# Turning a tile's hidden values in the middle of the results of the tile in front

## What is computed

```python
def _moe2_ref(x, expert_emb, tau, w1, w2):
    xn = x / (np.linalg.norm(x, axis=-1, keepdims=True) + 1e-06)
    en = expert_emb / (np.linalg.norm(expert_emb, axis=-1, keepdims=True) + 1e-06)
    logits = xn @ en.T / tau
    expert_idx = np.argmax(logits, axis=1)
    ...
    for e in range(E):
        mask = expert_idx == e
        h = np.maximum(x[mask] @ w1[e], 0.0)
        out[mask] = gate_w[mask, None] * (h @ w2[e])
```

## Time and profile before

| | us |
|---|---|
| median of 3 runs (lowest, highest) | 835.03 (833.4, 835.28) |
| the profiled execution | 834.27 |
| its span, first to last instruction | 832.3 |
| mean granted TensorE clock | 0.999 |
| TensorE busy (matmuls) | 814.6 (98%) |
| VectorE busy | 564.4 (68%) |
| ScalarE busy | 438.8 (53%) |
| GpSimd busy | 203.3 (24%) |

### The profile page before, as it was taken

One profiled execution on the slowest core, in us unless ns is written; L12 is line 12 of the kernel. 1 busy time (PEld: TensorE's weight loads), 2 busy tenths in 40 slices (PEclk: granted clock), 3 DMA queues, 4 the chain that ended last, 5 costly groups with the idle time before them and its releaser, 6 DMA issues.

```text
span 832.3 us, 18049 instructions
## 1 busy us (share of the span) xinstructions
PE 814.6 (98%) x5633; PEld 763.7 (92%) x5633; DVE 564.4 (68%) x1315; ACT 438.8 (53%) x924; POOL 203.3 (24%) x286
## 2 busy tenths in 40 slices
PE   6999999999999999999999999999999999999997
PEld 6899999999999999999999999999889998898896
DVE  6879788879889878879888855635452512545463
ACT  6675564464464465465456435553552533565563
POOL 5611111122103013103113001303343323334433
PEclk9999999999999999999999999999999999999999
DMA  9975432155242141232210001414531513376392
GB/s 215 206 150 130 77 68 39 34 92 69 51 73 34 31 84 33 39 83 38 39 34 30 1 16 30 171 47 128 168 124 40 185 47 100 134 259 201 92 315 66
DMA packets 165307, 78.56 MB, mean 94 GB/s; under 512 B 135486, under 2 KB 153253, under 8 KB 165090
## 3 DMA queue, kind: packets, MB, share of 16 engines
q1 hardware_dynamic: 156402, 64.81, 32.3%
q0 software_dynamic: 4544, 10.85, 4.0%
q10 hardware_dynamic: 4272, 1.82, 0.9%
HBM read 112.90 MB, written 11.63 MB: 150 GB/s over the span
## 4 chain that ended last, share of the span: by engine, by line
PE 85%; SPq 7%; DVE 3%; issue 2%; ACT 1%; DMA 1%; POOL 0%; DVEq 0%; ACTq 0%; POOLq 0%
PE bank L1065 22%; PE bank L1044 21%; PE bank L1117 13%; PE bank L1153 13%; SPq L458 3%; PE bank L1134 3%; PE bank L970 2%; PE bank L937 2%; PE bank L998 2%; PE bank L993 2%; SPq L483 1%; PE bank L1099 1%; PE bank L978 1%; SPq L471 1%; SPq L490 1%
## 5 line engine op out<-in xcount | busy, mean ns | idle before, releaser
L1044 PE MATMUL bank<-xhl,WRh 128*128 128x384 f32 x768 | 219.0, 339 | 0.7 <-DVE WRl L1715 0.5
L1044 PEld LDWEIGHTS bank<-xhl,WRh 128*128 128x128 f32 x768 | 141.3, 188 | 1.2 <-issue 1.2
L1411 ACT COPY gw<-bank 128x384 f32<-128x384 f32 x128 | 61.6, 481 | 152.3 <-PE bank L1044 150.9
L1065 PE MATMUL bank<-WRh,gh 128*128 128x384 f32 x384 | 135.8, 354 | 0.0
L1044 PE MATMUL bank<-xhl,WRl 128*128 128x384 f32 x384 | 130.0, 339 | 0.0
L1065 PE MATMUL bank<-WRh,gl 128*128 128x384 f32 x384 | 129.8, 338 | 0.0
L1065 PE MATMUL bank<-WRl,gh 128*128 128x384 f32 x384 | 129.7, 338 | 0.0
L1734 DVE TENSOR_TENSOR gl<-gw,gh 128x384 fp32r<-128x384 f32 x128 | 72.2, 564 | 56.6 <-ACT gh L1417 52.7
L1417 ACT CAST gh<-gw 128x384 fp32r<-128x384 f32 x128 | 65.2, 510 | 76.7 <-DVE gw L1727 64.4
L1727 DVE SCALAR_TENSOR_TENSOR gw<-gw 128x384 f32<-128x384 f32 x128 | 75.7, 592 | 31.3 <-ACT gw L1411 30.9
L1902 DVE TENSOR_TENSOR hl<-bank,hh 128x512 fp32r<-128x512 f32 x56 | 36.1, 686 | 84.0 <-ACT hh L1452 83.7
(11 more groups left out here) (199 smaller groups left out, 1639.7 us busy)
## 6 DMA issues: line engine op xcount, KB each, us to landing
stage<-in_moe_w_dram SPq DMA_DIRECT2D x96, 768.0 KB
Kn<-in_k_dram SPq DMA_DIRECT2D x24, 192.0 KB, 3.4
Vn<-in_v_dram SPq DMA_DIRECT2D x24, 192.0 KB, 3.2
x_moe<-x2s SPq DMA_DIRECT2D x24, 192.0 KB, 2.0
Rn<-in_r_dram SPq DMA_DIRECT2D x21, 192.0 KB, 2.8
wraw<-in_moe_w_out_dram SPq DMA_DIRECT2D x4, 768.0 KB, 7.4
eraw<-in_moe_w_dram SPq DMA_DIRECT2D x4, 768.0 KB, 8.9
Wn<-in_w_dram SPq DMA_DIRECT2D x152, 16.0 KB, 1.8
```

The lines of the kernel that those rows point to most:

```text
L1044: mm = pe.matmul(bank[F_BANK[n % 2]][:, 0:GN], win(t_)[:, f // 4, k_, cols], xhl[G % 2][:, a, k_, :], start=(k_ == 0 and n_ == 0), stop=(k ...
L1065: mm = pe.matmul(bank[O_BANK[i]][:, 0:DM], a[:, z, cols], wout(t_)[:, f, :], start=(f == 0 and n_ == 0), stop=(f == FT - 1 and n_ == 2))
L1411: act.copy(gw[:, n % 2, :], bank[F_BANK[n % 2]][:, 0:GN]).then_inc(s_g0, 1)
```

## The change

On TensorE the results of the tile in front are cut in two halves and the turns of tile j are put between them. The results of tile 0 (`start_moe`) and of the last tile keep their place. Which tile writes `s_o2`, and when, is as before: at the end of the second half. On ScalarE the rounding of the first half of tile j goes ahead of the scaled copy of tile j-1; that of the second half stays behind it.

```diff
             def result(j, s_):
+                result_half(j, s_, 0)
+                result_half(j, s_, 1)
+
+            def result_half(j, s_, a):
                 early_ = whole(j) and j < K1
                 _, (w2h, w2l) = views(eh, el) if early_ else expert(s_)
-                if not whole(j) or j > 1:
+                if a == 0 and (not whole(j) or j > 1):
                     pe.wait_ge(s_o2e, j - 1)
-                for a in range(2):
-                    pe.wait_ge(s_hhi, 2 * j + a + 1)
-                    pe.wait_ge(s_hlo, 2 * j + a + 1)
...
+                pe.wait_ge(s_hhi, 2 * j + a + 1)
+                pe.wait_ge(s_hlo, 2 * j + a + 1)
...
+                for f in range(4 * a, 4 * a + 4):
+                    for n_, (h_, w_) in enumerate(((hh, w2h), (hh, w2l), (hl, w2h))):
+                        mm = pe.matmul(bank[R_BANK[s_]][:, 0:DM], h_[:, f, :], w_[:, f, :],
+                                       start=(f == 0 and n_ == 0), stop=(f == FT2 - 1 and n_ == 2))
+                if a == 1:
+                    mm.then_inc(s_o2, 1)
 
             def tile(j, s_, half):
                 features(j, s_, half)
-                result(j - 1, 1 - s_)
+                result_half(j - 1, 1 - s_, 0)
                 turn_h(j)
+                result_half(j - 1, 1 - s_, 1)
...
                 if more_:
                     x_hi2(j + 1)
+                h_hi(j, 0)
                 scaled(j - 1, 1 - s_, half - 1 + s_)
-                h_hi(j, 0)
                 h_hi(j, 1)
```

More of the change, by code:

```diff
@@ L1137, in result @@
             def result(j, s_):
+                result_half(j, s_, 0)
+                result_half(j, s_, 1)
+            def result_half(j, s_, a):
                 early_ = whole(j) and j < K1
                 _, (w2h, w2l) = views(eh, el) if early_ else expert(s_)
-                if not whole(j) or j > 1:
+                if a == 0 and (not whole(j) or j > 1):
                     pe.wait_ge(s_o2e, j - 1)
-                for a in range(2):
-                    pe.wait_ge(s_hhi, 2 * j + a + 1)
-                    pe.wait_ge(s_hlo, 2 * j + a + 1)
[L1145 to L1155, removed]
+                pe.wait_ge(s_hhi, 2 * j + a + 1)
+                pe.wait_ge(s_hlo, 2 * j + a + 1)
+                if early_:
+                    pe.wait_ge(s_phi, a + 3)
+                    pe.wait_ge(s_plo, a + 3)
+                else:
+                    pe.wait_ge(s_ehi, 4 * (j - K1) + a + 3)
+                    pe.wait_ge(s_elo, 4 * (j - K1) + a + 3)
+                for f in range(4 * a, 4 * a + 4):
[4 more added lines that the diff above has]
+                    mm.then_inc(s_o2, 1)
             def tile(j, s_, half):
                 features(j, s_, half)
-                result(j - 1, 1 - s_)
+                result_half(j - 1, 1 - s_, 0)
                 turn_h(j)
+                result_half(j - 1, 1 - s_, 1)
             def mlp(first, lo, hi):
```

## The result

The changed kernel takes 841.9 us (median of five, 840.3 to 844.1) where the kernel before takes 834.41 (833.4 to 835.28): a ratio of 1.0095, 95% interval 1.008 to 1.011. That is 7.5 us more. The forecast was 838.5, with 840.4 as the upper end. A second series gave 840.28 (ratio 1.0061, 1.0047 to 1.0075), so the ten runs of this kernel lie around 841. The profiled execution is the longest of them, 844.1 us with a span of 842.0; before it was 834.27 and 832.3.

The account below looks back on a forecast made before the run. TensorE, always busy in the second MLP, was taken as the bound; 0.35 + 0.4 + 1.6 + 1.2 - 0.05 = +3.5 us gave 837.8 by the profile, 838.5 by the median, range 835.3 to 840.4.

Parts of the forecast that it names:

- What bounds the kernel, and which tiles are hit: Second MLP: TensorE always busy, so plain tiles stay 9.59 us; losses where weights are rounded ahead of late relus.
- one sign: Sign of being right: TensorE idle ahead of turns in tiles 20, 22 and 26 alone, about 0.8, 2.4, 1.2 us.
- the 2.08 us: Every tile: relus wanted 6.72 after the first feature matmul instead of 8.80, 2.08 us less time for ScalarE.
- The switch: TensorE's step from turns to matmuls, now results instead of features: 0.08 per tile either way, taken as zero.
- ScalarE's order: ScalarE in each tile: weights' roundings and relus behind them come 0.32 later after the first feature matmul.
- Tile 20: Four roundings in a row make relus late; TensorE stands 0.75, partly covered by the split-input wait: +0.4 us.
- Tile 22: Two roundings wait for DMA; weights and relus 1.2 later, TensorE stands about 2.45: +1.6 us, the largest term.
- Tile 26: Relus behind weight roundings come after the turns are wanted; TensorE stands uncovered: +1.2 us, bounds 0.8 and 1.8.
- Tile 5: VectorE's late split input holds the next features; called the same case as tile 20, 0.32 more: +0.35 us.
- The end: Last tile: gate column behind the scatter's drain bounds the last scaled copy; only 0.05 comes back: -0.05 us.
- TensorE's wait of 1.15: Ahead of the last tile's results TensorE waits for ScalarE and VectorE; with earlier turns this wait goes.
- waits feed each other: Rival: late turns shift next weights by more than TensorE itself; sum +5.4, 840.4 us, chance 0.13.

Follow-up runs that it names:

- e3: The whole change, with the relus and the input's rounding ahead of weight pieces 0 and 1 on ScalarE (VectorE likewise); 833.05 us, ratio 0.9987.
- e6: The change with the turns behind 18 of the 24 result matmuls instead of 12; 836.68 us, ratio 1.0022.
- e5: The changed kernel again, unaltered, for a second profile; 840.28 us.
- e2: ScalarE's new order alone on the kernel before, turns still behind the results; 836.27 us, ratio 1.0024.
- e7: The whole change, plus 12 extra TensorE matmuls into an unused bank ahead of the turns in tile 22 only; 838.52 us, ratio 1.0051.
- e11: The change, with GpSimd's drain and copies of token numbers and gate column ahead of the scatter; 843.89 us, ratio 1.0099.
- e4: The whole change, with SyncE's loads of a tile's weights ahead of the load of a token list; 841.59 us, ratio 1.0093.

## Why the prediction was wrong, by its own steps

- **What bounds the kernel, and which tiles are hit.** Right, but for one sign: TensorE has no slack in plain tiles, these still take 9.59, and the tiles that lost are the four of the sum. The prediction expected idle time ahead of the turns in tiles 20, 22 and 26 alone, and tile 5 had it too. e3 (relus on time) and e6 (turns wanted 1.05 later) bear out the 2.08 us as the main cause.
- **The switch.** Right: nothing in a plain tile. The excess of the first matmul moved from the features to the results.
- **ScalarE's order**, 0.32 later after F: right, 1.14 in tiles 5 and 26 where 0.83 was. In tile 21 ScalarE's weights start 1.28 after the first feature (758.85 against 757.57), forecast 1.15, before 0.37. What the same order does to GpSimd was left out, as said at tile 5.
- **Tile 20**: +0.4 forecast, +0.35 measured in the first profile, +1.05 in the second, where the fourth piece was 0.61 late for ScalarE.
- **Tile 22**: +1.6 forecast. Without a fall of the clock it was +1.75. The chain behind it (late weights of tile 21, VectorE, SyncE, DMA) was right: the relus start 8.34 after F, where it was 7.63 before and 8.43 in the forecast. With the fall it was +3.17.
- **Tile 26**: +1.2 forecast, +1.12 and +1.83. In the first profile the fourth piece was 0.97 late for ScalarE instead of 0.45.
- **Tile 5**: +0.35 forecast, +3.73 and +2.10 measured. This is the step that failed. It was costed as "the same case" as tile 20, with nothing put down for a late piece of its weights. The prediction asked of tile 22 what stands on SyncE ahead of the load, but not of tile 5, and nowhere what the scaled copy, now close ahead of the weights' roundings, does to GpSimd's copies. The runs showed the weights issued 3.63 us later and the fourth piece 1.7 to 2.1 late in four profiles (the change, e5, e2, e6), about 0.2 in two (e7, e11). In e4, where the piece is in time, the tile costs 0.31, about the forecast: what was left out is the late piece. The term is 1.75 us too small without a fall of the clock; with the fall it is 3.4 of the 6.2 us by which the first profile exceeds the forecast's +3.5.
- **The clock** is the term that was missing altogether: 1.6 us for each wait that ends in a fall. The prediction had turned a stall into time one for one. Two falls make 3.1 of the 9.7 us of the first profile.
- **The end**: -0.05 forecast, +0.59 and +0.8. The gate column bounds it as said, but it came 4.39 behind its scatter where 3.80 was taken over from the row. The sentence that TensorE's wait of 1.15 goes was wrong: the last tile's results start 1.19 us behind the last matmul in front of them (831.76 against 830.57, 0.85 of it shown as idle), though VectorE had finished their first half of inputs at 829.72. It is not the path that ends last, and what it is was not tried.

With the measured sizes in the order of tiles 20, 22, 26, 5 and the end, the sum is 0.3 to 1.1 + 1.8 + 1.1 to 1.8 + 2.1 + 0.6 to 0.8, 5.9 to 7.6, and falls of the clock in some executions; the ten runs lie 4 to 10 above the kernel before. That adds up two profiles and predicts nothing. Of the rivals, "waits feed each other" came nearest: its 2.0, 1.8 and 0.6 for tile 22, tile 26 and the end are about what was measured, and it too has tile 5 at 0.5.

## What to carry to other kernels

Moving a consumer forward in an engine's own order takes slack from every producer at once; look for the tiles in which a producer does its rare work (here the rounding of new weights) and compare its latest finish there with the new time of need. A move of half a microsecond on one engine has to be followed through the queues that wait for it until one is found with slack, for on the way it can be multiplied, as here where two small copies met two long remainders. Ahead of such a move, put the urgent small work in front of the rare large work: relus first gained 0.13 to 0.15% with either order of the turns, and with the gate column ahead of the scatter on the old order 0.23%. The intervals of these overlap, so none of them is shown to be the best.

## What was not expected of the hardware

- A wait of TensorE of about 2 us may cost 1.6 more, by the clock. Of the waits ahead of turns in these profiles, those of 1.67 us and less never ended in the lower level; of eight between 1.84 and 3.22 us six did (1.84, 2.20, 2.40, 2.41, 2.56, 3.22) and two did not (2.32, 2.34). So two profiles of the same kernel differ by 3.1 us in two tiles, and one profile of it isn't its typical run. The clock isn't all of the spread: of the ten runs, one at a mean granted clock of 0.999 took 841.9 and one at 0.996 took 839.87.
- A GpSimd copy of one column, 0.2 us alone, takes 1.7 to 1.8 us when it starts together with a VectorE remainder of 128x1536. The change did not invent this: in tile 20 of the kernel before, two such copies, at 749.26 and 750.92, already took 1.72 and 1.73 us under the remainders.
- The landing of a scatter of 0.2 MB at the end took 3.5 us before and 4.0 after, and all that stood behind the drain moved with it.
